# Attention, routing and two feed-forwards on one core: an earlier o_t copy, another order of the opening, and routing's constants moved behind attention's own work

## The reference

```
scores = q @ k^T / 8          # 2 batches, 8 heads, 768 tokens, 64 per head, float32
keep   = (key < 4) | (0 <= query - key < 128)          # 4 sinks and a window
a      = softmax(where(keep, scores, -1e9)) ;  x = (a @ v) as 1536 rows of 512
logits = x @ w_gate (8 experts); (token, expert) pairs in falling order of logit:
         a token takes the expert if it has none yet and the expert has under 192
y[t]   = relu(x[t] @ w1[e]) @ w2[e]
h      = y @ w_in;  out = (max(h,0) + alpha*min(h,0)) @ w_out
```

## Time and profile before

| | before |
|---|---|
| median of 3 runs | 665.18 us (664.56 to 667.4) |
| profiled execution | 667.12 us, span of the instructions 665.3 us |
| PE busy | 636.8 us (96%) |
| DVE, ACT, POOL busy | 420.6, 301.3, 200.5 us |
| mean granted TensorE clock | 0.987 of full speed |
| opening and slots 0 and 1 | 0 to 28.29 us |
| slots 2 to 11 | 28.29 to 112.15 us, 8.38 to 8.39 us each |
| slots 12, 13 | to about 121 us |

### The profile page before, as it was taken

One profiled execution on the slowest core, in us unless ns is written; L12 is line 12 of the kernel. 1 busy time (PEld: TensorE's weight loads), 2 busy tenths in 40 slices (PEclk: granted clock), 3 DMA queues, 4 the chain that ended last, 5 costly groups with the idle time before them and its releaser, 6 DMA issues.

```text
span 665.3 us, 12933 instructions
## 1 busy us (share of the span) xinstructions
PE 636.8 (96%) x4974; PEld 561.0 (84%) x4974; DVE 420.6 (63%) x1146; ACT 301.3 (45%) x704; POOL 200.5 (30%) x211
## 2 busy tenths in 40 slices
PE   7799999898999999999999999999999999999995
PEld 4688888546879988889999988899988889999994
DVE  6588887886659588864577789456587430035551
ACT  5677776102112464641226555323265551346662
POOL 8877772001011234212013422211034411113332
PEclk9799999898999999999999999999999999999998
DMA  7367754607062044006402330181034711000001
GB/s 249 144 210 266 250 196 141 223 7 269 5 225 100 1 174 151 1 2 222 152 1 83 117 127 1 49 274 53 1 128 125 248 59 45 1 0 1 1 0 48
DMA packets 31285, 72.37 MB, mean 109 GB/s; under 512 B 2940, under 2 KB 3000, under 8 KB 31224
## 3 DMA queue, kind: packets, MB, share of 16 engines
q1 hardware_dynamic: 27232, 60.69, 26.5%
q0 software_dynamic: 2048, 6.29, 3.1%
q10 hardware_dynamic: 1944, 4.56, 1.9%
HBM read 65.22 MB, written 6.32 MB: 108 GB/s over the span
## 4 chain that ended last, share of the span: by engine, by line
PE 87%; DVE 5%; ACT 2%; issue 2%; POOL 2%; DMA 1%; POOLq 0%; ACTq 0%; DVEq 0%
PE bank L1469 21%; PE bank L1480 20%; PE bank L1382 13%; PE bank L1373 13%; PE bank L1297 3%; PE bank L1216 3%; PE bank L1162 3%; DVE beats L857 2%; PE bank L1237 2%; PE bank L1145 2%; PE bank L1180 2%; DMA x_g<-x_rows,tok_next 1%; PE bank L1351 1%; PE bank L1329 1%; DVE neg_s L781 1%
## 5 line engine op out<-in xcount | busy, mean ns | idle before, releaser
L544 POOL TENSOR_TENSOR wi_lo<-w_in,wi_hi 128x512 fp32r<-128x512 f32 x64 | 86.3, 1351 | 278.0 <-ACT wi_hi L669 278.0
L857 DVE TENSOR_SCALAR beats<-rank_row,key 128x512 bf16<-128x512 f32 (+11 forms) x173 | 106.1, 637 | 20.0 <-PE bank L1299 19.9
L1480 PE MATMUL bank<-wo_hi,g_lo 128*128 128x512 f32 x192 | 76.0, 396 | 0.0
L1480 PE MATMUL bank<-wo_lo,g_hi 128*128 128x512 f32 x192 | 75.7, 394 | 0.0
L1480 PE MATMUL bank<-wo_hi,g_hi 128*128 128x512 f32 x192 | 75.4, 393 | 0.0
L1127 DVE SCALAR_TENSOR_TENSOR g<-bank,g_neg 128x384 f32<-128x384 f32 x64 | 35.5, 555 | 57.9 <-ACT g_neg L722 57.7
L720 ACT ACTIVATE g_neg<-bank 128x384 f32<-128x384 f32 x64 | 31.4, 491 | 78.8 <-PE bank L1469 78.8
L604 ACT ACTIVATE prob<-neg_s,neg_max 128x260 f32<-128x260 f32 x96 | 49.1, 512 | 26.4 <-DVE neg_max L781 25.6
L1469 PE MATMUL bank<-y_hi,wi_hi 128*128 128x384 f32 x256 | 58.5, 350 | 0.3 <-DVE g L1127 0.3
L695 ACT ACTIVATE h_t<-bank 128x192 f32<-128x192 f32 x64 | 21.2, 331 | 79.2 <-PE bank L1373 79.2
L1469 PE MATMUL bank<-y_hi,wi_lo 128*128 128x384 f32 x256 | 55.3, 337 | 0.0
(11 more groups left out here) (163 smaller groups left out, 1357.9 us busy)
## 6 DMA issues: line engine op xcount, KB each, us to landing
w_a<-moe_w SPq DMA_DIRECT2D x8, 1024.0 KB, 6.3
w_a<-moe_w SPq DMA_DIRECT2D x4, 2048.0 KB, 9.5
w_b<-moe_w SPq DMA_DIRECT2D x8, 1024.0 KB, 7.4
w_b<-moe_w SPq DMA_DIRECT2D x4, 2048.0 KB, 8.9
k_raw<-k_t SPq DMA_DIRECT2D x11, 512.0 KB, 4.8
q_raw<-q_t SPq DMA_DIRECT2D x11, 512.0 KB, 3.9
w_in<-moe_w_in SPq DMA_DIRECT2D x8, 512.0 KB, 5.3
w_out<-moe_w_out SPq DMA_DIRECT2D x8, 512.0 KB, 4.6
```

The source lines that it names most:

```text
L544: nc.gpsimd.tensor_tensor(out=wi_lo[:, f % 2, :, :], in0=w_in[:, :, f * P:(f + 1) * P], in1=wi_hi[:, f % 2, :, :].bitcast(F32), op=ALU.sub ...
L857: return nc.vector.tensor_scalar(out=beats[:, c % 3, lo:hi], in0=rank_row[:, lo:hi], scalar1=key[:, c:c + 1], scalar2=None, op0=op)
L1480: last = nc.tensor.matmul(DOWN_BANK[t][:, :], a[:, f % 3, t * P:(t + 1) * P], w[:, f % 2, :], start=(f == 0 and n == 0), stop=(f == FC - 1 ...
```

## The change

- ACT copies `o_t` behind head 1's exponential, no longer behind head 2's.
- Opening: 22 matmuls on zeros for 32. DVE takes head 0's maximum between the two halves of step 0's lower parts. ACT's `round_next_k(1)` stands ahead of slot 0 instead of behind head 0's exponential. `rest_of_q` of step 1 is DVE's, behind head 5's maximum in slot 0, instead of POOL's. PE's first score of a slot waits for `k_lo_done` too, and SP's load of step 3's k waits for it.
- POOL: `mask_even`, `mask_odd` and the routing's constants are made in slots 2, 4 and 6, behind the next step's lower parts.
- Step 0's sinks (`sinks_at`, slot 1): PE turns them behind head 4 (was 1) and multiplies them at head 7 (was 5); ACT's copy and DVE's split of them are at heads 5 and 6 (were 2 and 3).

```
+        def sinks_at(s):
+            return 1 if s else 4
...
             def load_k(s):
                 b, i = step(s)
+                if s == 3:
+                    sp.wait_ge(k_lo_done, 1)
...
-            build_mask(mask_even, 10, P, 0, True)
-            build_mask(mask_odd, 14, 0, P, True)
             pool.wait_ge(consts_ready, 2)
             nc.gpsimd.tensor_copy(turn_gate[:, :, 0:P], ...)
-            nc.gpsimd.memset(tri_before[:, :], 1.0).then_inc(consts_ready, 1)
...
+            def routing_consts():
+                nc.gpsimd.memset(tri_before[:, :], 1.0).then_inc(consts_ready, 1)
...
-                    rest_of_q(nc.gpsimd, nxt).then_inc(qk_split, 1)
+                    if nxt > 1:
+                        rest_of_q(nc.gpsimd, nxt).then_inc(qk_split, 1)
+                if s in (2, 4, 6):
+                    pool.wait_ge(qk_split, nxt)
+                if s == 2:
+                    build_mask(mask_even, 10, P, 0, True)
+                if s == 4:
+                    build_mask(mask_odd, 14, 0, P, True)
+                if s == 6:
+                    routing_consts()
                 if s == 0:
-                    pool.wait_ge(qk_split, 1)
                     pool.wait_ge(v_sinks_rounded, 1)
...
-                    if h == 0 and front + 1 < STEPS:
+                    if h == 0 and 1 < front + 1 < STEPS:
                         round_next_k(front + 1)
-                    if h == 2 and 0 <= end < STEPS:
+                    if h == 1 and 0 <= end < STEPS:
                         act.wait_ge(pv_done, 4 * (end + 1))
                         if end:
                             act.wait_ge(turned, 2 * end)
                         nc.scalar.copy(o_t[:, :, :], ...).then_inc(ot_copied, 1)
-                    if h == 2 and 0 <= mid < STEPS:
+                    if h == sinks_at(mid) + 1 and 0 <= mid < STEPS:
...
+            round_next_k(1)
             for s in range(STEPS + 2):
                 attention_slot(s)
...
+                    if front < STEPS and (s or h):
+                        head_max(front, h)
+                    if h == 5 and s == 0:
+                        dve.wait_ge(q_hi_done, 1)
+                        rest_of_q(nc.vector, 1).then_inc(qk_split, 1)
...
-                        if h == 3:
+                        if h == sinks_at(mid) + 2:
                             dve.wait_ge(st_copied, mid + 1)
...
                 rest_of_q(nc.vector, 0, heads).then_inc(qk_split_first, 1)
+                if n == 0:
+                    head_max(0, 0)
...
                         pe.wait_ge(qk_split, s)
+                        pe.wait_ge(k_lo_done, s)
...
-                    if h == 1 and 0 <= mid < STEPS:
+                    if h == sinks_at(mid) and 0 <= mid < STEPS:
                         turn_sinks(mid)
-                    if h == 5 and 0 <= mid < STEPS:
+                    if h == (5 if mid else 7) and 0 <= mid < STEPS:
                         sink_values(mid)
...
-            keep_clock(32, PT_BANK[0])
+            keep_clock(22, PT_BANK[0])
```

More of the change, by code:

```diff
@@ L459, in _ @@
             drop_sinks(mask_second, 9)
-            build_mask(mask_even, 10, P, 0, True)
-            build_mask(mask_odd, 14, 0, P, True)
             pool.wait_ge(consts_ready, 2)
             nc.gpsimd.tensor_copy(turn_gate[:, :, 0:P], ident[:, :].unsqueeze(1).to_broadcast([P, DC, P])).then_inc(consts_ready, 1)
-            nc.gpsimd.memset(tri_before[:, :], 1.0).then_inc(consts_ready, 1)
-            nc.gpsimd.memset(tri_after[:, :], -1.0).then_inc(consts_ready, 1)
-            affine(tri_before[:, :], ALU.is_gt, 0.0, [[1, P]], 0, -1, consts_ready, 4 + 2 + 1)
@@ L467, in _ @@
[L467 to L480, removed]
@@ L482, in _ @@
-            nc.gpsimd.iota(token_no[:, :], [[P, NT]], base=0, channel_multiplier=1,
-                           allow_small_or_imprecise_dtypes=True).then_inc(consts_ready, 1)
+            def routing_consts():
+                nc.gpsimd.memset(tri_before[:, :], 1.0).then_inc(consts_ready, 1)
+                nc.gpsimd.memset(tri_after[:, :], -1.0).then_inc(consts_ready, 1)
+                affine(tri_before[:, :], ALU.is_gt, 0.0, [[1, P]], 0, -1, consts_ready, 4 + 2 + 1)
+                affine(tri_after[:, :], ALU.is_gt, 0.0, [[-1, P]], 0, 1, consts_ready, 5 + 2 + 1)
+                nc.gpsimd.memset(ones[:, :], 1.0).then_inc(consts_ready, 1)
+                nc.gpsimd.memset(ones_row[:, :], 1.0).then_inc(consts_ready, 1)
+                nc.gpsimd.iota(slot_iota[:, :], [[1, CAP]], base=1, channel_multiplier=0,
+                               allow_small_or_imprecise_dtypes=True).then_inc(consts_ready, 1)
+                nc.gpsimd.iota(expert_no[:, :, :], [[0, NT], [-1, E]], base=E, channel_multiplier=0,
+                               allow_small_or_imprecise_dtypes=True).then_inc(consts_ready, 1)
+                nc.gpsimd.memset(full[:, :], 0.0).then_inc(consts_ready, 1)
+                nc.gpsimd.memset(full_pen[:, :], 0.0).then_inc(consts_ready, 1)
+                nc.gpsimd.memset(start_row[:, :, 0:E], 1.0 - CAP).then_inc(consts_ready, 1)
+                nc.gpsimd.memset(start_row[:, :, E], -2.0 * N).then_inc(consts_ready, 1)
+                nc.gpsimd.memset(free[:, :], 1.0).then_inc(consts_ready, 1)
+                nc.gpsimd.memset(cap_val[:, :], BIG).then_inc(consts_ready, 1)
+                nc.gpsimd.memset(assigned[:, :, :], 0.0).then_inc(consts_ready, 1)
+                nc.gpsimd.iota(token_no[:, :], [[P, NT]], base=0, channel_multiplier=1,
+                               allow_small_or_imprecise_dtypes=True).then_inc(consts_ready, 1)
@@ L767, in normalise, with head_max @@
                     in0=turned_blocks[:, :, 0:P].rearrange("p c (h d) -> p c h d", d=D), in1=factor(D), op=ALU.mult)
+            def head_max(s, h):
+                b, i = step(s)
+                n = H * s + h
+                if h == 0 and b == 0 and i < 4:
+                    dve.wait_ge(masks_ready, (5, 10, 14, 18)[i])
+                dve.wait_ge(scored, n + 1)
+                if n >= 4:
+                    dve.wait_ge(exped, n - 3)
+                which = (mask_first, mask_second)[i] if i < 2 else (mask_even, mask_odd)[i % 2]
+                nc.vector.tensor_tensor_reduce(
+                    out=neg_s[:, h % 4, :], in0=S_BANK[n % 3][:, 0:KW], in1=which[:, :],
+                    scale=-float(D) ** -0.5, scalar=BIG, op0=ALU.add, op1=ALU.min,
+                    accum_out=neg_max[b][:, h:h + 1]).then_inc(maxed, 1)
             def attention_slot(s):
```

## The result

The changed kernel takes 656.48 us (655.59 to 656.8, 4 runs) against 664.99 (664.56 to 667.4, 4 runs): 0.9863 of the time before, 95% interval 0.9837 to 0.9888. The forecast was 656.8 for 665.18. The profiled execution went from 667.12 to 656.8, its span from 665.3 to 655.1.

A forecast was written before the change was run, and what follows sets the result against it. Slot 2's start, set by POOL's queue, and the length of slots 2 to 11, with PE waiting for ACT's o_t copy, were taken as the bounds. -4.3 - 7.2 + 2.4 + 0.7 = -8.4 from 665.18 gives 656.8 us, range 653.8 to 662.0.

The forecast's parts named there:

- Slots: Attention slots 2 to 11: the earlier o_t copy removes PE's wait, 0.72 us a slot, -7.2 us in all.
- POOL's added work: Masks and constants in slots 2, 4 and 6 make PE wait 0.5, 0.5 and 1.4 us later: +2.4 us.
- Opening: Before slot 2: its start, set by POOL's queue, moves from 28.29 to 24.0 us, -4.3 us.
- (b): Opening, DVE: head 0's maximum between the halves pushes the second half's two instructions to about 10.8, 0.5 us later.
- (e): Opening: q's lower parts of step 1 on DVE take 1.3 us, 13.1 to 14.4; PE starts slot 1 at 14.45.
- The rule that I used for the masks: DVE instructions with two SBUF inputs contend with GpSimd ones reading SBUF; masks in the slots then cost 1.57 us each.
- bound of -3.3: Opening: the smaller end of the gain's range, -3.3 to -4.8 us, with v_sink_parts 1 us later.
- Clock: PE's gaps in the opening still bring a low-clock spell, costing in slot 2: +0.7 us, between 0 and 3.
- R4: The clock doesn't fall at all, the gaps being short: 656.1 us; its chance is within the forecast's 0.60.
- R1: Slots: a second chain (DVE's split or POOL's q_hl) takes over, only 0.50 a slot gained: 658.2 us, chance 0.19.
- R2: Slots hardly shrink because DVE or POOL comes later, 0.2 us gained each: 660.6 us, chance 0.13.
- R3: The clock stays low in the slots, 5.6 us lost a slot; with two slots 667.3 us, chance 0.06.

The follow-up runs named there:

- e1: The kernel before with one edit, ACT's o_t copy behind head 1's exponential instead of head 2's: 658.01 us, ratio 0.9873.
- e3: The changed kernel with mask_even and mask_odd made in the opening again and the routing's constants in slot 11: 654.53 us, ratio 0.9823.
- e2: The changed kernel with ACT's o_t copy back behind head 2's exponential: 662.01 us, ratio 0.9937.
- e4: The changed kernel with POOL's cast of step 1's q waiting until DVE has both halves of step 0 done: 656.59 us, ratio 0.9855.
- e7: The changed kernel with step 0's sinks turned behind head 1 and multiplied behind head 5 again: 657.39 us, ratio 0.9863.
- e5: e3 with the lower part of v_sink_parts made by DVE in slot 1 behind head 4's maximum instead of by POOL: 659.34 us, ratio 0.9900.
- e6: The changed kernel with q's lower part of step 1 on POOL again instead of DVE: 658.48 us, ratio 0.9886.
- e8: The changed kernel with 32 filler matmuls again instead of 22: 660.09 us, ratio 0.9911.
- e9: e3 with the lower part of v_sink_parts made by DVE in slot 0 behind head 7's maximum, in POOL's idle time: 655.09 us, ratio 0.9853.

## Why the prediction was right, step by step

The total was right, and so were the places and signs of the three parts. That it was right to 0.3 us is in part luck: the opening gained 0.9 less than forecast, POOL's work cost 0.6 less and the clock 0.7 less. Of the terms:

- **Slots: right, -7.2 forecast, -7.05 measured.** 0.72 a slot were forecast; a plain slot went from 8.39 to 7.65. The spacing, 0.66 and 0.10, was the right measure and the idle row's 0.50 was not: e1 shows 0.69 a slot on average. Slots 2, 4 and 6, whose first maximum has a wait for its mask in DVE's list, last 7.73 to 7.78 though POOL has nothing added there (e1 and e3; in e3 the masks were made long before, and still DVE's first maximum starts 0.65 behind PE's first score instead of 0.55). That is a term that I left out, 0.3 in all.
- **POOL's added work: right in mechanism and place, 2.4 forecast, 1.8 measured** (0.31, 0.36 and 1.12 for 0.5, 0.5 and 1.4; by e3 1.78 between the `turn_sinks`, 1.95 in the median). The masks took 1.57 each in their slots, the constants 2.34. That the cost hangs on the short slots is shown by e2, where it is zero.
- **Opening: right in mechanism, mis-sized: -4.3 forecast, -3.43 measured.** In the profiled execution the failed step is (b), "the second half's two instructions (0.7 to 0.88 and 0.69)": the second took 1.43. Everything behind it followed as worked out, 0.3 to 0.9 later: head 1's maximum at 11.44 (10.85), head 5's at 13.01 (12.7), slot 1 at 15.00 (14.45), v_sink_parts at 15.68 (14.8), slot 2 at 24.86 (24.0). But 24.0 wouldn't have come with (b) as forecast either: where the second half took 0.69 (e2, e3, e4, e7), step (e)'s 64x1024, put at 1.3, took 2.64 to 2.92 beside POOL's k_lo, POOL's v_sink_parts took 2.79 to 3.09 instead of 2.50, and slot 2 started at 24.52 to 24.86 (25.67 in e7, where PE's row decided). POOL's row from sink_p to q_hl lasted 6.44 (6.49). The rule that I used for the masks told of just this collision; I applied it to POOL's new work and not to DVE's beside POOL's cast. Its bound of -3.3 held.
- **Clock: wrong, and only partly known.** +0.7 was forecast, and in the profiled execution the granted clock stayed at 1.00 until behind attention (R4, to which 656.1 was given). The mean granted clock of the four runs is 0.994 in two and 0.991 in the other two (656.38 and 656.57 us), so the clock was low for longer in those, where isn't shown, and without a cost that shows. e2, with the same opening, had one in slot 2 that cost 1.5 us in its profiled execution. This error and the opening's nearly cancel: the parts as measured sum to -8.7, forecast -8.4.
- **R1, R2, R3.** R1 and R2 fall with e1. R3 didn't come; e2, e5, e6 and e8 show its mild form, slot 2 partly at the low clock, for 1.3 to 2.7 us in one execution each.

Not tried: undoing the maximum between the halves or the earlier `round_next_k(1)` alone, which of POOL's cast and k_lo would be better first in slot 0, and an earlier issue of q of step 1.

## What to carry to other kernels

What a wait is worth is read from the spacing of starts around it, compared with the same instructions where nothing waits, and not from its idle row: 0.74 us was gained here where the row said 0.50. Before work is moved out of a busy stretch, look whether its engine idles there for another reason (a load), and put it there or where the engine has no next step. Work that costs nothing in long slots can cost once they are shorter, so a gain and the work moved beside it have to be priced together. When a two-input tensor_tensor moves between VectorE and GpSimd, list what the other one reads from SBUF at that moment, and also if a load lands half a microsecond later, since the collision can cost more than the instruction.

## What the runs showed of the hardware that I had not expected

- A DVE tensor_tensor with both inputs in SBUF that began while POOL was in a cast or a tensor_tensor of its own was held until that one's end: 2.21 for 0.69 beside one k_lo (e8); 2.92 for 1.22 (e4 and e8, 64x1024); 1.43 for 0.69 beside a cast (after). The 64x1024 one ended 1.08 us behind the end of POOL's k_lo both in the changed kernel (13.86 to 14.94) and in e4 (14.58 to 15.66), though it had begun 2.0 us into k_lo in the one and 0.5 into it in the other. Of the two in e5, 5.53 us where e9 needs 1.29, each took 2.8: one ended 0.6 behind the end of POOL's k_lo, the other 0.55 behind the end of its q_hl. The other way round POOL lost less: 3.09 for 2.53, 1.19 for 1.04. The Trainium skill (SBUF — State Buffer, Who interferes with whom) says that the two contend; the trace agrees, with these delays. DVE's maxima, with one input in PSUM, kept 0.43 us beside the same work of POOL's.
- The clock's fall was not settled by the length of PE's last gap alone. At the start of slot 1 PE had been idle for 2.31 us in e4 and 2.04 in e7 and e9, and the granted clock fell to 0.50 within slot 1 (in e7 behind a second gap, of 1.83); it had been idle for 2.20 us in e3 and 2.03 in e2, and the clock stayed at 1.00 through slot 1.
